# Five token groups in place of six in a dense stage in split fp32, with the finished rows kept in spent input columns

## What is computed

```python
def _moe2_ref(x, w_in, w_out):          # x: 2304 x 512, w_in: 512 x 2048, w_out: 2048 x 512
    h = x @ w_in
    g = np.where(h >= 1, h, np.where(h <= -1, 0.0, (h + 1) ** 2 / 4.0))
    return (g @ w_out).astype(np.float32)
```

## Time and profile before

| what | value |
|---|---|
| median of 3 runs | 740.69 us (739.46 to 742.4) |
| the profiled execution's own time | 742.33 us |
| its span in the profile | 740.5 us |
| TensorE busy with matmuls, share of the span | 93% |
| VectorE, ScalarE, GpSimd busy | 52%, 33%, 20% |
| granted TensorE clock, mean over the span | 0.97 of full speed |

### The profile page before, as it was taken

The page is one execution under the profiler, slowest core; times in us unless marked ns, Lnnn a source line. Parts: engine busy times, 40 slices in busy tenths (PEclk is TensorE's granted clock), DMA queues, the critical chain, the costliest instruction groups (busy, mean ns, idle before and its releaser), DMA issues.

```text
span 740.5 us, 11427 instructions
## 1 busy us (share of the span) xinstructions
PE 691.9 (93%) x4000; PEld 635.4 (86%) x4000; DVE 381.5 (52%) x833; ACT 247.3 (33%) x749; POOL 151.3 (20%) x165
## 2 busy tenths in 40 slices
PE   7999999029999999989999999999999999999995
PEld 4898889029999999978889998999999989989994
DVE  5999962804211122158656555645655474556543
ACT  4999972103111111112323223322322232233221
POOL 4445420730222222478001000100010010001001
PEclk9999999659999999989999999999999999999998
DMA  8655426469277777534001000100010010001001
GB/s 234 181 167 131 139 85 257 159 219 401 78 261 261 260 260 260 175 89 112 1 1 44 0 1 1 42 0 0 0 42 0 0 42 0 0 0 43 0 0 43
DMA packets 38814, 73.87 MB, mean 100 GB/s; under 512 B 3075, under 2 KB 16292, under 8 KB 38772
## 3 DMA queue, kind: packets, MB, share of 16 engines
q1 hardware_dynamic: 35900, 63.91, 26.8%
q0 software_dynamic: 2880, 9.52, 3.2%
HBM read 63.48 MB, written 9.94 MB: 99 GB/s over the span
## 4 chain that ended last, share of the span: by engine, by line
PE 89%; POOL 3%; DVE 2%; ACT 2%; DMA 2%; issue 1%; SPq 1%; DVEq 0%
PE bank L944 27%; PE bank L957 26%; PE bank L902 10%; PE bank L912 10%; PE bank L802 4%; PE bank L824 4%; POOL x_sorted L403 3%; PE bank L854 2%; PE bank L812 2%; PE bank L798 1%; PE bank L886 1%; ACT xrow L497 1%; DMA k_loc<-kT 1%; ACT prob L475 1%; DMA xfirst<-x_sorted 0%
## 5 line engine op out<-in xcount | busy, mean ns | idle before, releaser
L554 ACT ACTIVATE cl<-cl,half 128x384 f32<-128x384 f32 x96 | 59.2, 617 | 191.7 <-DVE cl L761 191.7
L957 PE MATMUL bank<-WOH,gl 128*128 128x512 f32 x288 | 113.8, 395 | 0.0
L957 PE MATMUL bank<-WOL,gh 128*128 128x512 f32 x288 | 113.6, 395 | 0.0
L957 PE MATMUL bank<-WOH,gh 128*128 128x512 f32 x288 | 112.3, 390 | 0.9 <-DVE gl L769 0.9
L769 DVE TENSOR_TENSOR gl<-gr,gh 128x384 fp32r<-128x384 f32 x96 | 59.2, 617 | 70.4 <-ACT gh L563 70.4
L464 POOL DMA_INDIRECT out<-rows_out,tok x18 | 17.3, 963 | 365.0 <-DVE rows_out L749 361.4
L761 DVE TENSOR_SCALAR cl<-bank 128x384 f32<-128x384 f32 x96 | 53.4, 556 | 66.4 <-PE bank L944 66.4
L944 PE MATMUL bank<-yl,WIH 128*128 128x384 f32 x384 | 85.1, 341 | 1.7 <-DVE yl L741 1.7
L944 PE MATMUL bank<-yh,WIH 128*128 128x384 f32 x384 | 84.3, 341 | 0.9 <-ACT yh L532 0.9
L944 PE MATMUL bank<-yh,WIL 128*128 128x384 f32 x384 | 82.8, 336 | 0.0
L563 ACT CAST gh<-gr 128x384 fp32r<-128x384 f32 x96 | 49.3, 514 | 85.2 <-PE bank L957 62.1
(11 more groups left out here) (112 smaller groups left out, 877.1 us busy)
## 6 DMA issues: line engine op xcount, KB each, us to landing
WE<-w SPq DMA_DIRECT2D x16, 2048.0 KB, 11.7
xrow<-x_sorted SPq DMA_DIRECT2D x6, 781.5 KB, 10.6
raw_in<-win SPq DMA_DIRECT2D x16, 256.0 KB, 9.4
raw_out<-wout SPq DMA_DIRECT2D x16, 256.0 KB, 2.6
v_loc<-vl SPq DMA_DIRECT2D x4, 768.0 KB, 4.5
q_str<-qT SPq DMA_DIRECT2D x4, 576.0 KB, 4.9
k_str<-kT SPq DMA_DIRECT2D x8, 288.0 KB, 5.9
q_loc<-qT SPq DMA_DIRECT2D x3, 576.0 KB, 4.7
```

The source lines that it names most:

```text
L554: act.activation(cl[:, :], cl[:, :], ACT.Square, bias=half[:, :], scale=0.5).then_inc(squared, 1)
L957: last = pe.matmul(fin_b[t][:, :], x[:, f % 2, P * t:P * (t + 1)], w[:, f, :], start=(f == 0 and k == 0), stop=(f == FFC - 1 and k == 2))
```

## The change

`G` goes from 384 to 512: four groups of 512 tokens (`FULL` = 4, `GT` = 4 tiles) and one of 256 (`REST`, 2 tiles). The sort ahead of the experts keeps its pieces of 384 tokens, now called `SORTED`. `up` has 12 matmuls of 512 columns (256 in the last group), `down` has 12 of 512 columns (6 in the last group), and `fin_b` has four banks. `finish` copies tiles 0 and 2 on VectorE and 1 and 3 on ScalarE.

`rows_out` is gone: a finished tile is written into columns of `XT` that the group has used up (`rows_of`), and the last group's two tiles into those of group 0, behind a wait for group 0's output DMAs (`first_out_done`). The wait of each `finish` for the output DMAs of the group before is gone with it. The rounded buffers lie in the order `yl`, `gh`, `yh` over the experts' `hid`, `xw` and `gb`; `warm` shares their place.

TensorE has group 0 straight, three groups in a loop and the last straight; ScalarE and VectorE have groups 0, 3 and 4 straight and two in a loop.

```diff
-G = 384
-NG, GT = N // G, G // P
+SORTED = 384
+NS, ST = N // SORTED, SORTED // P
+G = 512
+FULL, GT = N // G, G // P
+REST = N - FULL * G
...
-        yh, _, o = at("yh", [P, DC, G], F32R, h_at)
-        yl, _, o = at("yl", [P, DC, G], F32R, o)
+        yl, _, o = at("yl", [P, DC, G], F32R, h_at)
         gh, _, o = at("gh", [P, 2, G], F32R, o)
-        rows_out, _, o = at("rows_out", [P, GT, D], F32, o)
+        yh, _, o = at("yh", [P, DC, G], F32R, o)
...
-        h2_b, fin_b = bank[6:8], bank[0:3]
+        h2_b, fin_b = bank[6:8], bank[0:4]
...
+        def rows_of(g, t):
+
+            return XT[:, t, bass.ds(0 if isinstance(g, int) and g == FULL else G * g, D)]
...
-                    pool.indirect_dma_start(out, bass.IndirectOffsetOnAxis(tok[:, GT * g + t:GT * g + t + 1], 0), rows_out[:, t, :], None).then_inc(out_done, 16)
-            pool.wait_ge(out_done, 16 * NT)
+            for g in range(FULL + 1):
+                for t in range(GT if g < FULL else REST // P):
+                    pool.wait_ge(fin_act if t % 2 else fin_dve, GT // 2 * g + t // 2 + 1)
+                    pool.indirect_dma_start(out, bass.IndirectOffsetOnAxis(tok[:, GT * g + t:GT * g + t + 1], 0), rows_of(g, t), None).then_inc(out_done if g else first_out_done, 16)
+            pool.wait_ge(first_out_done, 16 * GT)
+            pool.wait_ge(out_done, 16 * (NT - GT))
...
-            def finish(g):
-                for t in (0, 2):
+            def finish(g, tiles=GT):
+                for t in range(0, tiles, 2):
                     dve.wait_ge(fin_tile, GT * g + t + 1)
-                    behind(dve, out_done, 16 * GT * g)
-                    dve.tensor_copy(rows_out[:, t, :], fin_b[t][:, :]).then_inc(fin_dve, 1)
+                    if isinstance(g, int) and g == FULL:
+                        dve.wait_ge(first_out_done, 16 * GT)
+                    dve.tensor_copy(rows_of(g, t), fin_b[t][:, :]).then_inc(fin_dve, 1)
...
-                        last = pe.matmul(h2_b[f % 2][:, 0:G], w[:, c, P * f:P * (f + 1)], x[:, c, :], start=(k == 0), stop=(k == 3 * DC - 1))
+                        last = pe.matmul(h2_b[f % 2][:, 0:tokens], w[:, c, P * f:P * (f + 1)], x[:, c, 0:tokens], start=(k == 0), stop=(k == 3 * DC - 1))
...
-                for t in range(GT):
+                for t in range(tokens // P):
...
-            group(0)
-            with pe.Fori(1, NG) as g:
-                group(g)
-            down(NG - 1, FFC - 1)
+            group(0, G)
+            with pe.Fori(1, FULL) as g:
+                group(g, G)
+            group(FULL, REST)
+            down(FULL, FFC - 1, REST)
```

More of the change, by code:

```diff
@@ L525, in _, with highs @@
                     relus(E + i, 1)
-            def highs(g):
+            def highs(g, n=G):
                 for c in range(DC):
@@ L531, in highs, with group @@
                         act.wait_ge(y_added, DC * (E - 1 + more_n) + c + 1)
-                    act.copy(yh[:, c, :], XT[:, c, bass.ds(G * g, G)]).then_inc(y_high, 1)
+                    act.copy(yh[:, c, 0:n], XT[:, c, bass.ds(G * g, n)]).then_inc(y_high, 1)
             highs(0)
-            def finish(g):
[L538 to L543, removed]
+            def finish(g, tiles=GT):
+                for t in range(1, tiles, 2):
+                    act.wait_ge(fin_tile, GT * g + t + 1)
+                    if isinstance(g, int) and g == FULL:
+                        act.wait_ge(first_out_done, 16 * GT)
+                    act.copy(rows_of(g, t), fin_b[t][:, :]).then_inc(fin_act, 1)
+            def group(g, n, following):
                 for f in range(FFC):
-                    n = FFC * g + f
+                    k = FFC * g + f
                     if f == 1 and not (isinstance(g, int) and g == 0):
                         finish(g - 1)
-                    if f == FFC - 1 and not last:
+                    if f == FFC - 1 and following:
                         act.wait_ge(h2_ready, FFC * (g + 1))
[L551 to L555, removed]
+                        highs(g + 1, following)
+                    act.wait_ge(clamped, k + 1)
+                    act.activation(cl[:, 0:n], cl[:, 0:n], ACT.Square, bias=half[:, :], scale=0.5).then_inc(squared, 1)
+                    act.wait_ge(g_ready, k + 1)
                     if f == 1:
@@ L562, in group @@
                         act.wait_ge(wi_low, FFC)
[L563 to L569, removed]
+                    act.copy(gh[:, f % 2, 0:n], gr[:, 0:n]).then_inc(g_high, 1)
+            group(0, G, G)
+            with act.Fori(1, FULL - 1) as g:
+                group(g, G, G)
+            group(FULL - 1, G, REST)
+            group(FULL, REST, 0)
+            finish(FULL, REST // P)
         @block.vector
@@ L743, in _, with finish @@
             lows(0)
-            def finish(g):
-                for t in (0, 2):
+            def finish(g, tiles=GT):
+                for t in range(0, tiles, 2):
                     dve.wait_ge(fin_tile, GT * g + t + 1)
-                    behind(dve, out_done, 16 * GT * g)
-                    dve.tensor_copy(rows_out[:, t, :], fin_b[t][:, :]).then_inc(fin_dve, 1)
-            def group(g, last):
+                    if isinstance(g, int) and g == FULL:
+                        dve.wait_ge(first_out_done, 16 * GT)
+                    dve.tensor_copy(rows_of(g, t), fin_b[t][:, :]).then_inc(fin_dve, 1)
@@ L771, in _ @@
[L771 to L775, removed]
+                    if f == FFC - 1 and following:
+                        lows(g + 1, following)
+                    dve.wait_ge(h2_ready, k + 1)
+                    behind(dve, g_ready, k)
+                    dve.tensor_scalar(cl[:, 0:n], h2_b[f % 2][:, 0:n], -1.0, 1.0, ALU.max, ALU.min).then_inc(clamped, 1)
+                    behind(dve, g_low, k)
@@ L777, in _ @@
+            group(0, G, G)
+            with dve.Fori(1, FULL - 1) as g:
+                group(g, G, G)
+            group(FULL - 1, G, REST)
+            group(FULL, REST, 0)
+            finish(FULL, REST // P)
         @block.tensor
@@ L931, in _, with up @@
                     outof(E + i, 1, E // 2 + 1 + i)
-            def up(g, f):
+            def up(g, f, tokens):
                 n = FFC * g + f
```

67 lines of the change are left out of this document (30 added, 37 removed).

## The result

The changed kernel takes 732.53 us (median of 4 runs, 731.74 to 733.13), the kernel before, timed beside it, 741.55 us (median of 4). The ratio is 0.988, with a 95% interval of 0.9852 to 0.9909. The forecast was 731 us, the range 728.5 to 737.

A forecast was written before the change was run, and what follows sets the result against it. TensorE, busy 93% of the span, was taken as the bound. Terms of -7.5, -1.9, +0.2, 0 and -0.6 summed to -9.8 us: 732.5 for the profiled execution, 731 us as median, range 728.5 to 737.

The forecast's parts named there:

- The stream of matmuls: Dense stage on TensorE: 192 fewer up matmuls at 13.3 ns fixed cost, no up-down step cost in full groups: -7.5 us.
- Group 0: First chunks beside the weight splits: TensorE's 5.44 us a chunk outlasts two GpSimd rounds, so the stall goes: -1.9 us.
- Start: Dense stage's beginning: longer wait for the four yl, less bigger matmuls done within it: +0.2 us, between -0.3 and +0.8.
- Between groups: Group boundary: chunk 15 takes 7.3 us after up(15), TensorE needs it after 8.2 us, so 0.
- Tail: After the last matmul: two output tiles instead of three, last DMA starts 1.98 us behind instead of 2.56: -0.6 us.
- The sum: All terms for the whole kernel: -7.5 - 1.9 + 0.2 - 0.6 = -9.8 us, giving a median of 731 us.
- the pairs of full groups: Rival, full groups: each up-down pair still costs 67 ns, -5.8 us in all, 735 us; chance 0.27.
- the last group's narrow matmuls: Rival, last group: up matmuls take 173 ns, not 120, +10 us, 741; milder form, VectorE bounds, +3, 734; chance 0.06.
- the boundary: Rival, between full groups: chunk 15 comes late, TensorE waits and the clock falls, 747 us; chance 0.03.
- The clock: Rival, dense stage's start: bigger matmuls fill the waits, the clock stays up, -2.3 us, 729 us; chance 0.08.

The follow-up runs named there:

- the hold from the fifth split on: Changed kernel, GpSimd's output-weight splits from the fifth on held until group 0's first gl: 729.81 us; also with TensorE's high-part products first: 728.10 us.
- three later variants: Changed kernel with the first two ups' yh products first, 730.69 us; with output-weight splits held from the fifth on, 729.81 us; with both, 728.10 us.
- a fourth: Changed kernel with the first two ups' yh products first and GpSimd's last eight output-weight splits held until group 0's second gl: 730.71 us.

## Why the prediction was right, point by point

- **The stream of matmuls** (forecast -7.5): both parts held. 87.04 us a full group is the forecast's number; one shape costs nothing from kind to kind, at 512 and at 384, and four columns of difference bring the cost back. The 13.3 ns a matmul held at 256 columns. In the last group a pair cost 20 ns, not 67, which is 0.7 us better.
- **Group 0** (forecast -1.9): right against the profiled execution of before, where the stall is 1.88 us, but two things in its reason were off. "VectorE's round for one chunk (two such instructions) is tied to two GpSimd rounds" holds in the profiles of before (4.66 us) and after (4.78), not in general: at 384 tokens, with other buffers, VectorE ran ahead in rounds of 3.4 to 4.0 us, and the two tied rounds that came then cost nothing. And "nothing is lengthened" with 512 tokens did not come true: `gl` takes 1.70 us there too. The stall is gone because TensorE needs 5.44 us and the tied round 4.78. (The 4.54 us for two GpSimd rounds came from a single round of 2.27; seven rounds of before, from 335.56 to 351.78, average 2.32, so two are 4.63.) That the two engines keep each other waiting was shown by the start: 4.40 us beside GpSimd, 2.50 without. How much of the 1.9 us a median of the kernel before contains stays open. In seven profiles with full groups of 512 columns (the changed kernel and its variants that keep this shape) every down and up of group 0 from the second down on took 2.72 us.
- **Start** (forecast +0.2): from the first matmul to the first down it went from 12.81 us to 14.96, +2.15; 36 matmuls of 53.3 ns more are 1.92 of it, so +0.23. The `yl` grew by 0.95 us, within the bounds given. That it fits so closely is luck: with the same instructions the four `yl` took 4.40 to 5.24 us in the eight profiles at 512 tokens without the hold from the fifth split on, 3.45 to 4.61 in the four at 384, and in the changed kernel without the last eight subtractions the first down came 16.70 us after the first matmul.
- **Between groups** (forecast 0): right. 6.7 us against the 7.3 allowed for, and 8.2 to be had.
- **Tail** (forecast -0.6): the last DMA starts 0.59 us closer to the last matmul. What follows it took 0.2 us more in this execution (725.17 to 731.4, against 734.46 to 740.5), so 0.4 came through.
- **The sum:** from the first dense matmul to the last 409.65 us became 399.92, -9.7, where the forecast's terms without the tail make -9.2. The dense stage began 1.0 us later in this execution (in the fourteen profiles it began between 321.6 and 324.6 us), and with the tail the span is 9.1 us shorter. The forecast was -9.8. The medians differ by 9.0 us. The changed kernel's came out 1.6 us above 740.69 - 9.8 = 730.9, 0.9 of it because the kernel before took 741.55 us beside the changed one and not 740.69.
- **The rivals:** the pairs of full groups cost nothing (2.72 us for each kind), the last group's narrow matmuls stood 119 to 120 ns apart and its pair took 2.82 us, so neither form of that rival came, and the boundary did not run dry. The clock fell at the start as before. It stayed up in three later variants that left TensorE less idle there, which is what that rival had as its condition, but it fell in a fourth that did so too; what decides stays open.

## What to carry to other kernels

When one matmul follows the other without a wait, take the distance between starts at two widths from the trace and split it into a part for the columns and a fixed part; the fixed part times the matmuls saved is the gain. Look for steps between runs of different shapes too: here that cost, invisible in any list of waits, was twice as large as the fixed part, and a row of the same trace with one shape told that it would go. Before holding work back to free a port, count in the timeline which instance of it really runs there.

## What the runs showed of the hardware

- A float32r matmul with 128x128 weights stands at (columns + 32) cycles of 2.4 GHz from the next: 226.7 ns at 512, 173.3 at 384, 120 at 256 (24 of them on end take 2.87 us). At 1.2 GHz the 32 cycles didn't show: the matmuls of 384 columns in the slow stretch of before stand 320 ns apart (four start at 329.58 and the next four at 330.86 us in the timeline of before).
- A change of the moving width, even from 512 to 508, makes some of the matmuls behind it slower, up to nine of them (in the kernel before, a down of nine takes 2.08 us behind an up and 2.04 behind a down): 0.02 to 0.07 us for a pair of changes. Why is open.
- VectorE's two-input instructions and GpSimd's subtractions wait for each other in either order (1.68 us instead of 0.56 on VectorE, 1.65 instead of 1.29 on GpSimd). The Trainium skill (SBUF — State Buffer, on the shared port pair) says that whichever starts first holds it for the whole instruction; the trace agrees. That this is also why two kernels with the same work in group 0 ran with a stall in one's profile and without in the other's is likely, but not shown.
